# Sliding-window attention with sinks, SoLU and a gated expert stack on one core: x rounded and subtracted earlier in a pair, and the first weight segment in another place of GpSimd's queue

## The reference

```python
scores = scale * q @ k.T                       # kept where sink or in the window
a = exp(scores - max(scores)); a = a / (sum(a) + 1e-9)
x = a @ v                                      # 1536 x 512 over all heads
h = x @ w_in                                   # 1024 wide
e = exp(h - max(h)); solu = h * e / (sum(e) + 1e-9)
y = layer_norm(solu) * g_ln @ w_out
gate = softmax(y @ w_gate), divided by row and column sums eight times
out = sum over e of gate[:, e] * (relu(y @ w1[e]) @ w2[e])
```

## Time and profile before

| | |
|---|---|
| median of three runs | 1252.02 us |
| profiled execution | 1253.09 us, its span 1251.3 us |
| busy, of the span | PE 99%, DVE 55%, POOL 43%, ACT 29% |
| first product of the MLP begins | at 93.88 us |
| issue of the first segments on SyncE | 7.19 us (w_in) and 7.59 us (w_out); landed 4.0 and 4.3 us on |
| GpSimd from `normalise(0, 1)` to `round_segments(0)` | 10.25 us to 11.81 us |

### The profile page before, as it was taken

One profiled execution on the slowest core, in us unless ns is written; L12 is line 12 of the kernel. 1 busy time (PEld: TensorE's weight loads), 2 busy tenths in 40 slices (PEclk: granted clock), 3 DMA queues, 4 the chain that ended last, 5 costly groups with the idle time before them and its releaser, 6 DMA issues.

```text
span 1251.3 us, 18785 instructions
## 1 busy us (share of the span) xinstructions
PE 1236.2 (99%) x6446; PEld 1097.3 (88%) x6446; DVE 691.7 (55%) x1348; ACT 365.1 (29%) x832; POOL 535.7 (43%) x625
## 2 busy tenths in 40 slices
PE   7999999999999999999999999999999999999998
PEld 4558899989988999999999999999999999999997
DVE  7895734356665555555555555555555555555554
ACT  7884634312233222222222222222222222222221
POOL 7772315644444444444444444444444444444440
PEclk9999999999999999999999999999999999999999
DMA  6440000111110111111111111111111111111102
GB/s 204 156 149 18 1 1 1 34 35 34 34 35 28 38 36 36 34 34 34 34 34 34 34 34 34 34 34 34 34 34 34 34 34 34 34 34 34 35 18 101
DMA packets 57264, 53.13 MB, mean 42 GB/s; under 512 B 4352, under 2 KB 44544, under 8 KB 57216
## 3 DMA queue, kind: packets, MB, share of 16 engines
q1 hardware_dynamic: 56928, 52.19, 13.1%
q10 hardware_dynamic: 288, 0.33, 0.1%
HBM read 49.35 MB, written 3.15 MB: 42 GB/s over the span
## 4 chain that ended last, share of the span: by engine, by line
PE 95%; ACT 2%; DVE 2%; DMA 1%; issue 1%; SPq 0%; DVEq 0%; ACTq 0%
PE ps L797 30%; PE ps L798 30%; PE ps L799 30%; PE ps L722 2%; PE ps L766 1%; PE ps L742 1%; PE ps L847 1%; ACT probs L1042 1%; ACT acc L1218 1%; DVE probs L1270 1%; DMA k_sb<-kT 0%; PE ps L977 0%; DVE xw L1303 0%; ACT xw L1066 0%; DMA q_sb<-qT 0%
## 5 line engine op out<-in xcount | busy, mean ns | idle before, releaser
L1528 DVE SCALAR_TENSOR_TENSOR acc<-ps,gate_now,acc 128x512 f32<-128x512 f32 x336 | 252.1, 750 | 166.2 <-PE ps L799 162.0
L797 PE MATMUL ps<-ring 128*128 128x512 f32 x768 | 300.6, 391 | 0.0
L798 PE MATMUL ps<-ring 128*128 128x512 f32 x768 | 299.8, 390 | 0.0
L799 PE MATMUL ps<-ring 128*128 128x512 f32 x768 | 299.2, 390 | 0.0
L1200 ACT ACTIVATE sums<-ps 128x384 f32<-128x384 f32 x192 | 94.4, 492 | 597.8 <-PE ps L799 597.8
L1504 DVE TENSOR_TENSOR sums<-ps,sums 128x384 f32<-128x384 f32 x192 | 106.9, 557 | 158.2 <-ACT sums L1200 106.9
L799 PEld LDWEIGHTS ps<-ring 128*128 128x128 f32 x768 | 144.3, 188 | 30.9
L797 PEld LDWEIGHTS ps<-ring 128*128 128x128 f32 x768 | 144.2, 188 | 27.9 <-DVE acc L1524 0.4
L798 PEld LDWEIGHTS ps<-ring 128*128 128x128 f32 x768 | 144.2, 188 | 25.8
L642 POOL TENSOR_TENSOR w_raw<-w_raw 128x256 f32<-128x256 f32 x32 | 23.7, 741 | 321.3 <-PE ps L799 321.3
L797 PE MATMUL ps<-xw,ring 128*128 128x384 f32 x448 | 152.5, 340 | 0.3 <-ACT sums L1200 0.2
(11 more groups left out here) (148 smaller groups left out, 1765.2 us busy)
## 6 DMA issues: line engine op xcount, KB each, us to landing
w_in<-w_exp SPq DMA_DIRECT2D x64, 256.0 KB, 3.2
w_raw<-w_exp SPq DMA_DIRECT2D x64, 128.0 KB, 2.8
w_raw<-w_exp SPq DMA_DIRECT2D x32, 256.0 KB, 3.2
v_sb<-v SPq DMA_DIRECT2D x16, 192.0 KB
out<-acc SPq DMA_DIRECT2D x12, 256.0 KB, 2.0
q_sb<-qT SPq DMA_DIRECT2D x7, 384.0 KB, 4.4
k_sb<-kT SPq DMA_DIRECT2D x7, 384.0 KB, 4.9
k_sb<-kT SPq DMA_DIRECT2D x9, 256.0 KB, 5.7
```

The costliest lines, as they stand in the source:

```text
L797: pe.matmul(o, ws[0], xs[0], start=first, stop=False, skip_group_check=True)
L798: pe.matmul(o, ws[0], xs[1], start=False, stop=False, skip_group_check=True)
L799: return pe.matmul(o, ws[1], xs[0], start=False, stop=last, skip_group_check=True)
L1528: dve.scalar_tensor_tensor(out=acc[:, T, :], in0=y_bank(u, T), scalar=gate_now[:, T:T + 1], in1=acc[:, T, :], op0=ALU.mult, op1=ALU.add).t ...
```

## The change

Three edits, all in the attention stage, none of which adds or takes away an instruction.

ScalarE: `round_x(p - 2)` goes from behind the first two exponentials of pair `p` to ahead of them, and `scale_probs(p - 1, 2)` goes one tile on, behind the exponentials of tile 1.

VectorE: `normalise(p - 1, 2)`, `rest_x(p - 2)` and `copy_pT(p - 1, 1, 1)` go from behind the masks of tile 0 to behind those of tile 1, and the rest of x is now the first of the three.

GpSimd, pair 0 alone: `round_segments(0)` goes ahead of `normalise(0, 1)`, and `rest_w_out(0)` goes behind `normalise(0, 2)` and `split_sinks(0)`.

```diff
@@ GpSimd
             for p in range(PAIRS):
                 normalise(p, 0)
-                if p > 0:
+                if p == 0:
+                    round_segments(0)
+                else:
                     rest_w_in(p)
                 normalise(p, 1)
                 if p + 1 < PAIRS:
                     lay_sinks(p + 1)
                 if p == 0:
-                    round_segments(0)
                     rest_w_in(0)
-                rest_w_out(p)
+                else:
+                    rest_w_out(p)
                 if p == 4:
                     rest_router()
                 normalise(p, 2)
                 split_sinks(p)
+                if p == 0:
+                    rest_w_out(0)
                 round_v_sinks(p)
@@ ScalarE
             def back(p, t):
 
-                if t == 0 and p > 1:
-                    round_x(p - 2)
                 if t == 0 and p > 0:
                     copy_pT(p - 1, 1, 0)
+                if t == 1 and p > 0:
                     scale_probs(p - 1, 2)
...
             for p in range(PAIRS):
+                if p > 1:
+                    round_x(p - 2)
                 for t in range(QT):
...
+            round_x(PAIRS - 2)
             back(PAIRS, 0)
+            back(PAIRS, 1)
             exp_h(0)
@@ VectorE
             def back(p, t):
 
-                if t == 0 and p > 0:
-                    normalise(p - 1, 2)
+                if t == 1 and p > 0:
                     if p > 1:
                         rest_x(p - 2)
+                    normalise(p - 1, 2)
                     copy_pT(p - 1, 1, 1)
...
-            back(PAIRS, 0)
+            back(PAIRS, 1)
```

## The result

| | median | profiled span | mean clock granted to TensorE, as a share of full speed |
|---|---|---|---|
| before | 1252.03 us (1251.76 to 1252.48, 4 runs) | 1251.3 us | 1.000 |
| changed | 1285.62 us (1285.10 to 1289.34, 4 runs) | 1283.3 us | 0.984 |

The ratio is 1.027 (95% interval 1.0257 to 1.0283): 33.6 us slower, where 6.7 were predicted.

A forecast was written before the change was run, and what follows sets the result against it. PE is busy from the MLP's start, so only that start counts: k at 26.9, C of pair 2 at 31.7, five pairs of 11.92 and 9.27 put it at 100.6, 6.7 later: 1258.7 us (8 in 10: 1253.0 to 1259.6).

The forecast's parts named there:

- the meeting of L1297 and L565: Each steady pair: VectorE's rest of v's sinks falls 0.02 behind GpSimd's rest of w_in and waits it out; pairs of 11.92.
- I let L1285 wait: VectorE's scaling in each steady pair waits for GpSimd's rounding L556 (0.62) and ends 0.15 later.
- a lead of 0.05: VectorE's scaling starting up to 0.05 ahead of GpSimd's instruction was taken to lose its turn, from a scaling that took 0.81.
- rival A: L1297 just ahead of L565, or L1285 not held up: pairs of 11.10, 1253.5 us, no change to be told; chance 0.27.
- GpSimd's edit: Pair 0: SyncE's issue goes to 18.8 and k of pair 2 lands 8.16 later, at 26.9: costs 3.2 us (2.5 to 3.7).
- No rest of x waits for ScalarE: Sign in pairs 3 to 7: VectorE's rest of x no longer waits for ScalarE's rounding.
- The loop without a stop: A steady pair of the attention stage, if nothing new stops it, takes 11.10 us against about 11.5 before.

The follow-up runs named there:

- e4: The changed kernel with sixteen transposes of the identity, into columns that nothing reads, where TensorE waits ahead of tile 5's scores: 1275.50 us.
- e14: The changed kernel with GpSimd's rounding of v's sinks (L527) on all 128 rows instead of 72: 1257.61 us.
- e2: The changed kernel with GpSimd's order as before, so only the orders of ScalarE and VectorE changed: 1282.77 us.
- e11: The kernel before with the changed ScalarE and VectorE orders, and from pair 1 all GpSimd work on the segments later: 1257.57 us.
- m2: VectorE and GpSimd alone, running the kernel's whole sequence with the 72-row rounding: VectorE's scaling took 3.31 to 3.73 us in 13 of the first 18 arrivals.
- m3: The m2 sweep with GpSimd's small rounding on 72, 128 or 64 rows, left out, or behind the large roundings; one 128-row cell took 0.65 against 3.39.
- e3: The changed kernel with GpSimd's two roundings of a segment behind its scaling of batch 0 in every pair: 1258.76 us.
- e8: The changed kernel with GpSimd's scaling of batch 0 waiting for VectorE's in pairs 2 to 7, which makes a gap behind L559: 1262.91 us.
- m1: VectorE and GpSimd alone, 80 arrivals of a VectorE instruction against gapless GpSimd work without the 72-row rounding: the 128x128 scaling took 0.49 us in the mean.
- e15: The kernel before with the changed ScalarE and VectorE orders, and GpSimd's rounding of v's sinks on 128 rows: 1253.43 us.

## Why the prediction was wrong

Slower was right, its size was not, and the step that carried most of the forecast, the meeting of L1297 and L565, never took place. So that the direction held is in part luck. By its own steps:

**The sum of the result.** From k of pair 2 to the MLP: 100.1 us in the changed kernel, 88.2 with TensorE kept busy, 71.6 with the seams open, 70.2 before. So the 32.1 us are 11.9 of clock, 16.6 of closed seams (six waits of 3.39 - 0.65 = 2.74 make 16.4), 2.2 of the later k, and 1.4 that is left for the x orders' own path and the clock behind k. The 11.9 are shown by e4, which takes the low clock away and leaves the seams closed. No run opens the seams and keeps the low clock behind them, so the 16.6 are the difference of e4 and e14, and the six waits make the check. By e14 alone the two together are 28.5; by the medians it gives back 28.0.

**The step that failed: "I let L1285 wait: L556 takes 0.62, the scaling ends 0.15 later".** The place was right to 0.1 (0.04 behind the start of L556 in all six; VectorE needed 0.51 from the inverse sums to the scaling, not 0.41), the victim and the blocker too. The price was that of one instruction, 0.77, and it was that of five, 3.39. All waits in the rows of before end with the instruction in flight, and I took that for a rule. What they have in common I hadn't looked at: none lies behind the 72-row rounding L527 without a gap between. The one wait in the attention stage of the kernel before that does (the inverse sums of pair 2 at 29.93, 0.47) meets a gap of GpSimd's where L559 ends, so it couldn't tell. In the changed kernel GpSimd goes from L543 to L565 without a gap, and VectorE comes in behind L527.

**The rule of the Trainium skill.** The Trainium skill ("SBUF — State Buffer", Who interferes with whom) says that whoever issues first has the shared pair for the whole instruction and the other is blocked. By that the wait would have ended at 35.69. The runs say otherwise behind an instruction on 64 or 72 rows: the wait went on over five of GpSimd's instructions, each of them on all 128 rows. Which engine is served at a lead of 0.05 wasn't put to the test here, since VectorE came 0.04 behind. The prediction read it from a scaling of 260 columns that lost with such a lead (57.27, 0.81 us). The scaling of 128 columns that it was about had kept its turn in the same trace with the same lead to 0.01 (30.65 above, 0.29 us; GpSimd's L517 followed at 30.70).

**The meeting of L1297 and L565.** It never took place in the changed kernel, since VectorE was held until L565 was over (L1304 took 0.28). With the seams open (e14) it went the other way than forecast: VectorE came 0.08 ahead, not 0.02 behind, and kept its turn. So this step was wrong in its own right, by 0.1 in a sum of eight rows, as rival A said: GpSimd's side was right (L557 + 2.09), and VectorE's was L557 + 2.01 for 2.11, since the scaling of 128 columns ends 0.07 behind L557 and not 0.15.

**The clock.** The prediction had no term for it: it put the clock at nothing without a reason. Each step that let TensorE idle was counted at the length of the wait. But 2.01 us of wait in a pair came with 2.0 us of slow matmuls behind it (11.9 over six).

**GpSimd's edit.** SyncE's issue was forecast for 18.8 and came at 18.81. k was forecast for 26.9, and came at 25.91 (25.06 to 28.20 in the ten other runs with the same edit), 7.1 behind the issue and not 8.16. Alone the edit cost 5.9, not 3.2: k was 3.5 later in that run, and the time from k on grew by 2.7 at the low clock, with `normalise(1, 0)` behind the late segment in GpSimd's queue. The prediction followed SyncE's queue past the moved step, and not GpSimd's.

**What held.** No rest of x waits for ScalarE any more, and the product is released by it. The loop without a stop was put at 11.10 (11.12 with the two exponentials at the 1.00 that their rows give, not 0.98), and runs with open seams gave 11.25 to 11.36. The range ended at 1259.6 because I bounded the wait from above by the one instruction that I knew.

## What to carry to other kernels

Where VectorE and GpSimd share SBUF, don't price a wait of one by the instruction in flight alone: list GpSimd's instructions back to back around it, and look for one on fewer than 128 rows ahead. A helper that works on a few rows is better run on all 128, where the others hold nothing that matters, or put where a gap follows; e14 got 28 us back that way, with 128 rows for 72. And a stall can cost TensorE twice, once as idle time and again as matmuls at half clock: the six stalls of 2.01 us did, while one of 1.59 (e2) and one of 1.86 (e11) did not. So look at the granted clock behind each stall before saying what it is worth.

## What the runs showed of the hardware that I had not expected

- A GpSimd instruction on 64 or 72 rows keeps VectorE out of the seams behind it until GpSimd has a gap or is done: 3.26 to 3.73 us against 0.29 to 0.65 with 128 rows, with both engines alone (m2, m3), and 3.39 against 0.65 in the kernel (e14). Other numbers of rows weren't tried, and by what means it does so stays open, as does the one place in e3 (59.73) where VectorE got in without a gap.
- It holds for VectorE's scaling by a column and for an instruction with two inputs (3.39 and 3.46), and ends at the first gap (e8, a gap of 0.23 us; a gap of 0.06 right behind the 72-row instruction was enough in e3).
- Without such an instruction VectorE gets in at the next seam, or where GpSimd's last instruction ends, at all 80 arrivals of m1 (0.28 to 0.78 us, two seams tried); where it comes within about 0.05 of the seam it is the one after.
- TensorE's clock was 0.50 from about 40 to 46.8 us behind 2 us of idleness (37.5 to 39.5), and full where sixteen transposes filled them. Behind a wait for k of 1.6 us it was 0.50 for 3.4 us in e15 and stayed at 1.00 in e2.
